# A fused attention and gated-MLP kernel: weight pieces are loaded before the first q and k, and their splitting is moved ahead

## The reference

```python
def _moe_ref(x, w1, w2, w3, w_out):
    a = x @ w1                      # 512 -> 1024
    b = x @ w2
    h = a * b @ w3                  # 1024 -> 1024
    return h @ w_out                # 1024 -> 512

def _moe2_ref(x, w1, w2, w3, w_out):
    h = np.maximum(np.maximum(x @ w1, x @ w2), x @ w3)   # 512 -> 768
    return h @ w_out                                     # 768 -> 512
```

## Time and profile before

| | us |
|---|---|
| median of 3 runs | 704.42 |
| lowest and highest run | 702.22, 706.07 |
| the profiled execution, whole | 706.01 |
| its span | 704.2 |
| TensorE busy in the span | 684.6 |
| mean granted TensorE clock | 0.995 |

### The profile page before, as it was taken

The page is one execution under the profiler, slowest core; times in us unless marked ns, Lnnn a source line. Parts: engine busy times, 40 slices in busy tenths (PEclk is TensorE's granted clock), DMA queues, the critical chain, the costliest instruction groups (busy, mean ns, idle before and its releaser), DMA issues.

```text
span 704.2 us, 15733 instructions
## 1 busy us (share of the span) xinstructions
PE 684.6 (97%) x6632; PEld 608.6 (86%) x6632; DVE 376.4 (53%) x705; ACT 242.2 (34%) x514; POOL 264.5 (38%) x241
## 2 busy tenths in 40 slices
PE   6999999999999999999999988999999999999998
PEld 4777788888888888888887988999999999999997
DVE  3464554414544044432665646566775667746673
ACT  5364432313332233333655544122341223403221
POOL 6799432312234023231222129043490434903341
PEclk9999999999999999999999998999999999999999
DMA  9874222111222022103998979876589765797632
GB/s 322 274 227 145 65 84 76 56 43 55 76 77 76 24 76 76 55 25 110 312 309 288 332 263 373 291 247 238 182 299 379 248 240 179 302 369 253 214 132 90
DMA packets 43798, 131.73 MB, mean 187 GB/s; under 512 B 4944, under 2 KB 8272, under 8 KB 42960
## 3 DMA queue, kind: packets, MB, share of 16 engines
q1 hardware_dynamic: 43728, 130.73, 53.7%
HBM read 103.97 MB, written 26.74 MB: 186 GB/s over the span
## 4 chain that ended last, share of the span: by engine, by line
PE 82%; DMA 6%; DVE 4%; POOL 3%; ACT 2%; issue 1%; SPq 1%; ACTq 0%; DVEq 0%
PE psum L585 25%; PE psum L587 24%; PE psum L586 24%; DMA weights_stream<-attention 4%; PE psum L624 2%; PE psum L602 2%; PE psum L595 2%; DVE attention L749 2%; POOL second_split L1147 2%; ACT attention L993 2%; DMA attention<-qk 2%; PE psum L612 1%; PE psum L633 1%; SPq L534 1%; DMA xy<-wa 1%
## 5 line engine op out<-in xcount | busy, mean ns | idle before, releaser
L585 PE MATMUL psum<-second_split,weights_split 128*128 128x384 f32 x402 | 135.7, 338 | 4.3 <-POOL second_split L1147 2.9
L586 PE MATMUL psum<-second_split,weights_split 128*128 128x384 f32 x402 | 134.9, 336 | 0.0
L587 PE MATMUL psum<-second_split,weights_split 128*128 128x384 f32 x402 | 134.9, 336 | 0.0
L1147 POOL TENSOR_TENSOR second_split<-xy,second_split 128x384 fp32r<-128x384 f32 x75 | 81.9, 1119 | 133.6 <-ACT second_split L993 133.6
L1147 POOL TENSOR_TENSOR h_split<-gate,h_split 128x512 fp32r<-128x512 f32 (+1 forms) x40 | 47.1, 1177 | 205.3 <-ACT h_split L993 205.3
L585 PE MATMUL psum<-x_split,weights_split 128*128 128x512 f32 (+1 forms) x320 | 120.4, 376 | 0.0
L587 PE MATMUL psum<-x_split,weights_split 128*128 128x512 f32 (+1 forms) x320 | 117.9, 369 | 0.0
L586 PE MATMUL psum<-x_split,weights_split 128*128 128x512 f32 (+1 forms) x320 | 117.9, 368 | 0.0
L585 PEld LDWEIGHTS psum<-second_split,weights_split 128*128 128x128 f32 x402 | 76.0, 189 | 6.6 <-issue 3.9
L586 PEld LDWEIGHTS psum<-second_split,weights_split 128*128 128x128 f32 x402 | 75.9, 189 | 0.0
L587 PEld LDWEIGHTS psum<-second_split,weights_split 128*128 128x128 f32 x402 | 75.9, 189 | 0.0
(11 more groups left out here) (101 smaller groups left out, 1152.5 us busy)
## 6 DMA issues: line engine op xcount, KB each, us to landing
weights_split<-weights_stream SPq DMA_DIRECT2D x39, 768.0 KB, 5.2
weights_split<-weights_stream SPq DMA_DIRECT2D x54, 512.0 KB, 5.0
weights_stream<-attention SPq DMA_DIRECT2D x48, 256.0 KB, 3.1
xy<-wa SPq DMA_DIRECT2D x40, 256.0 KB, 4.9
attention<-qk SPq DMA_DIRECT2D x16, 576.0 KB, 4.2
weights_stream<-attention SPq DMA_DIRECT2D x24, 384.0 KB, 2.8
weights_split<-weights_stream SPq DMA_DIRECT2D x6, 1152.0 KB, 5.0
attention<-v_win SPq DMA_DIRECT2D x16, 384.0 KB, 3.6
```

What stands on the lines that cost most here:

```text
L585: pe.matmul(out, lhs[:, 0], rhs[:, 0], start=first, stop=False, skip_group_check=read_between)
L586: pe.matmul(out, lhs[:, 0], rhs[:, 1], start=False, stop=False, skip_group_check=read_between)
L587: return pe.matmul(out, lhs[:, 1], rhs[:, 0], start=False, stop=last, skip_group_check=read_between)
L1147: return pool.tensor_tensor(out, full, high.bitcast(F32), ALU.subtract)
```

## The change

Seven edits, all in the first 40 us:

1. SyncE issues pieces 0 and 1 ahead of q and k of unit 0, then pieces 2 and 3 and the mask. Then it waits until q and k have landed, and issues the rest.
2. S of unit 0 moves behind step 3 of W3O, and T, V and S of the next unit follow: TensorE's order becomes steps 0 to 3, S, steps 4 to 10, T, steps 11 to 14, V, steps 15 and 16, S of unit 1, steps 17 to 23, T, steps 24 to 31, V. From there on the order is the old one.
3. Pieces 0 to 15 are split nine positions ahead of their slab's steps, not five. ScalarE therefore splits pieces 0 to 7 before the exponentials of unit 0, and pieces 12 and 13 before, 14 and 15 right behind those of unit 1. The positions at which pieces 12 to 27 are loaded stay as they were (`REFILL`), but q and k of unit 1 move with S of unit 0 and now stand behind pieces 16 and 17.
4. Steps 0 to 3 run term by term: four matmuls high by high, four high by low, four low by high, each term with its own wait.
5. The lows of pieces 1 and 3 are made by VectorE (`early_low`), with a semaphore of their own, and not by GpSimd.
6. VectorE fills 128 columns of `gate` with zeros, and TensorE multiplies them eight times (fp32, 128 columns) before step 0.
7. The semaphore on which TensorE and SyncE wait for a low of w3 is chosen by `wait_w3`.

```diff
-FIRST_VISITS = {"S": [-0.5, 15, 34.5, 47.5], "T": [7, 22, 40.7, 53.7], "V": [12, 31.9, 45.3, 58.3]}
+FIRST_VISITS = {"S": [3.5, 16.5, 34.5, 47.5], "T": [10, 23.5, 40.7, 53.7], "V": [14, 31.9, 45.3, 58.3]}
...
+EARLY = 2
+AHEAD, REFILL = 9, 5.5
...
-        out += [(4 * k - 5, ("SPLIT", 2 * k)), (4 * k - 4.9, ("SPLIT", 2 * k + 1))]
+        out += [(4 * k - AHEAD, ("SPLIT", 2 * k)), (4 * k - AHEAD + 0.1, ("SPLIT", 2 * k + 1))]
...
-    out = [(at + 1.5, ("PIECE", step[1] + SLOTS)) for at, step in weight_splits() if step[1] + SLOTS < PIECES]
+    out = [(at + (REFILL if step[1] < 2 * F1 else 1.5), ("PIECE", step[1] + SLOTS)) for at, step in weight_splits() if step[1] + SLOTS < PIECES]
...
-            load_qk(0)
             load_piece(0)
             load_piece(1)
+            load_qk(0)
             load_piece(2)
+            load_piece(3)
             sp.dma_start(mask, mask_in).then_inc(const_in, 16)
-            load_piece(3)
-            load_v4(0)
+
+            sp.wait_ge(qk_in, 16)
             load_piece(4)
             load_piece(5)
+            load_v4(0)
             sp.dma_start(ident, ident_in).then_inc(const_in, 16)
-            load_v(0)
             load_piece(6)
             load_piece(7)
+            load_v(0)
...
+            def first_product(i):
+
+                if i:
+                    return
+                high, both = (lambda i: w3_tile(0)[:, 0, P * i:P * (i + 1)]), w_out_tile(0)
+                pe.wait_ge(w_out_hi, 1)
+                pe.wait_ge(w3_hi, 1)
+                for i in range(4):
+                    pe.matmul(bank(i), high(i), both[:, 0], start=True, stop=False)
+                pe.wait_ge(w_out_lo, 1)
+                for i in range(4):
+                    pe.matmul(bank(i), high(i), both[:, 1], start=False, stop=False)
+                wait_w3(pe, 0)
+                for i in range(4):
+                    pe.matmul(bank(i), w3_tile(0)[:, 1, P * i:P * (i + 1)], both[:, 0], start=False,
+                              stop=False).then_inc(w3o_step, 1)
...
+            pe.wait_ge(zeros_made, 1)
+            for i in range(WARM):
+                pe.matmul(bank(7)[:, 0:P], gate[:, 0, 0:P], gate[:, 0, 0:P], start=True, stop=True)
...
+            def early_low(m):
+                dve.wait_ge(w3_hi, m + 1)
+                low(w3_tile(m)[:, 1, :], stage_a[2 * m + 1], w3_tile(m)[:, 0, :]).then_inc(w3_lo_early, 1)
+
+            dve.memset(gate[:, 0, 0:P], 0.0).then_inc(zeros_made, 1)
...
-                                 product_out(), after_parts("H"),
+                                 product_out(), after_parts("H"), [((-3.5, -2.5)[m], ("EARLY_LOW", m)) for m in range(EARLY)],
...
+            of_vector = [("SPLIT", 2 * m + 1) for m in range(EARLY)]
```

More of the change, by code:

```diff
@@ L48 @@
 SLOTS = 12
+WARM = 8
+EARLY = 2
+AHEAD, REFILL = 9, 5.5
 ATT = 6104
@@ L386, in build @@
         stage_a = [xy[:, T * (i // 3) + S + 512 * (i % 3):T * (i // 3) + S + 512 * (i % 3 + 1)] for i in range(SLOTS)]
-        const_in = sem("const_in")
+        const_in, zeros_made = sem("const_in"), sem("zeros_made")
         qk_in = sem("qk_in")
@@ L396, in build @@
         w_out_hi, w_out_lo = sem("w_out_hi"), sem("w_out_lo")
-        w3_hi, w3_lo = sem("w3_hi"), sem("w3_lo")
+        w3_hi, w3_lo, w3_lo_early = sem("w3_hi"), sem("w3_lo"), sem("w3_lo_early")
         w12_hi, w12_lo = sem("w12_hi"), sem("w12_lo")
@@ L426, in ge, with wait_w3 @@
                 eng.wait_ge(semaphore, value)
+        def wait_w3(eng, m):
+            if m < EARLY:
+                eng.wait_ge(w3_lo_early, m + 1)
+            else:
+                eng.wait_ge(w3_lo, m - EARLY + 1)
         def w3_tile(m):
@@ L496, in load_piece @@
                     elif kind == "w3":
-                        sp.wait_ge(w3_lo, n + 1)
+                        wait_w3(sp, n)
                     else:
@@ L635, in values @@
                 mm.then_inc(down_filled, 1)
+            def first_product(i):
[13 more added lines that the diff above has]
+                              stop=False).then_inc(w3o_step, 1)
             def product(half, k, i):
                 m = F1 * half + k
+                if m == 0:
+                    first_product(i)
+                    return
                 if i == 0:
-                    pe.wait_ge(w3_lo, m + 1)
+                    wait_w3(pe, m)
                     if half == 0:
@@ L859, in make_y @@
                 add.then_inc(y_made, 1)
-            run = {"qk_sum": qk_sum, "down_max": down_max, "local_max": local_max, "scale_down": scale_down,
+            def early_low(m):
+                dve.wait_ge(w3_hi, m + 1)
+                low(w3_tile(m)[:, 1, :], stage_a[2 * m + 1], w3_tile(m)[:, 0, :]).then_inc(w3_lo_early, 1)
+            dve.memset(gate[:, 0, 0:P], 0.0).then_inc(zeros_made, 1)
+            run = {"EARLY_LOW": early_low, "qk_sum": qk_sum, "down_max": down_max, "local_max": local_max, "scale_down": scale_down,
                    "scale_local": scale_local, "x_out": x_out, "W3O_OUT": product_low,
@@ L1183, in _ @@
                    "E": lambda e, kp: split_y(0, e, kp)}
-            for step in in_order(unit_jobs(["v_sum"]), weight_splits(), x_splits(), after_parts("H"),
+            of_vector = [("SPLIT", 2 * m + 1) for m in range(EARLY)]
+            for step in in_order(unit_jobs(["v_sum"]), [x for x in weight_splits() if x[1] not in of_vector],
+                                 x_splits(), after_parts("H"),
                                  [x for x in first_activations(0.4) if x[1][0] == "E"]):
```

## The result

The kernel after has a median of 706.53 us (702.66 to 707.93, 22 runs); the kernel before, run on the same chips, 703.38 us (702.22 to 707.72, 22 runs). The ratio is 1.0032 with a 95% interval of 1.0018 to 1.0045, some 2.3 us. (The means are 705.98 and 703.76, 2.2 apart; the medians lie 3.15 apart.) That is within the 0.5% that I called no change, but it is a small loss and not nothing. Its profiled execution has a span of 706.1 us (before 704.2) and a mean granted clock of 0.993. Neither profiled execution is a typical one: that of the kernel after, 707.93 us in all, is the longest of its 22, and that of the kernel before, 706.01, lies 2.6 above its median.

A forecast was written before the change was run, and what follows sets the result against it. TensorE, busy 684.6 of 704.2 us, was taken as the bound, leaving only its waits to gain. Landing later +2.5, shorter way -2.5 and clock +1.1 gave +1.1 us: median 705.5, range 701.3 to 707.6.

The forecast's parts named there:

- Step 0 near 5.4: Start of the kernel: piece 0 lands at 4.0, piece 1 at 4.8, so step 0 starts at about 5.4 us.
- rival 4: Start: piece 0 still takes 4.03 us, step 0 starts at 6.2, the end stays at 705.5; chance 0.07.
- q and k of unit 0 at 6.6: Start: this load, now third, lands at 6.6 us (range 6.0 to 7.4), just in time for S of unit 0.
- T of unit 0 with a wait of 1.4 at 16.4: Behind step 10: T can't start before some 16.4 us, TensorE is there at 14.9, a new wait of 1.4.
- q and k of unit 1 at 24.6, bounds 22.9 and 25.5: Load now behind pieces 16 and 17: leaves at about 14.6, lands at 24.6 us, 2.5 later than before.
- A wait of 3 to 4.5 before S of unit 1: TensorE, there at 23.0 or so, waits 3 to 4.5 us; S of unit 1 starts at 26.8.
- The issue wait goes: Scores of unit 1: TensorE's wait of 1.2 us for its own instructions probably goes, since S comes later.
- From S of unit 1 to step 28: 10.4 and 1.1 for the clock: This stretch takes 10.4 us, 12.93 before; one spell at half clock behind the long wait adds 1.1.
- The zeros are undone before S of unit 1: Eight zero matmuls at the start: by the skill's rule, the long wait before S of unit 1 undoes them.
- A shift passes to the end one to one: Behind the prologue everything is ordered behind TensorE, so a shift of the prologue reaches the end unchanged.
- Rival 2's cap: q and k of unit 1 not pushed back: step 28 up to 4.5 us earlier, 699.9 to 703.5; chance 0.23.
- Rival 3: SyncE's wait for the low of piece 5 makes q and k of unit 1 land after 27.0: 708 to 711; chance 0.07.

The follow-up runs named there:

- e2: Kernel after without SyncE's wait for q and k of unit 0; 706.14 us, ratio 1.0037 to the kernel before.
- e6: Kernel after without the matmuls of zeros; 705.04 us, ratio 1.0029 to the kernel before.
- e7: Kernel after with the lows of pieces 1 and 3 made by GpSimd, not VectorE; 705.22 us, ratio 1.0032 to the kernel before.
- e1: Kernel after with q and k of unit 1 issued right behind piece 11, ahead of pieces 12 to 17; 705.44 us, ratio 1.0026 to the kernel before.
- e10: e8 without the matmuls of zeros; 701.68 us, ratio 0.9971 to the kernel before.
- e12: e8 with q and k of unit 0 issued first again, ahead of pieces 0 and 1; 703.64 us, ratio 1.0004 to the kernel before.
- e8: Kernel after without SyncE's wait, q and k of unit 1 behind piece 11, pieces 12 and up held until V of unit 0 has run; 701.65 us, ratio 0.9978.
- e11: e8, but only pieces 12 to 15 go behind v of unit 1, the rest behind q and k of unit 2; 701.63 us, ratio 0.9971.
- e3: Kernel after without SyncE's wait and with q and k of unit 1 right behind piece 11; 704.28 us, ratio 1.0007 to the kernel before.
- e4: Kernel before with q and k of unit 1 issued right behind piece 11; 703.46 us, ratio 0.9994 to the kernel before.
- e9: Kernel before with q and k of unit 1 behind piece 11 and pieces 12 and up held until V of unit 0 has run; 702.77 us, ratio 0.9994.

## Why the prediction was right, and where not

The forecast, that q and k of unit 1 land later and eat the gain, holds by its main steps. I said 1.1 us slower; measured is 2.3 (1.3 to 3.2), so the size was too small by a factor of two. That the time itself, 706.53, comes near my 705.5 is in part luck: I started from a median of three runs, 704.42, and 22 runs of the same kernel give 703.38. Point by point:

- **Step 0 near 5.4.** It was 4.82. Piece 0 landed 2.7 us after its issue, not in the 4.03 that it had before; rival 4, no earlier step 0, is out. Both loads in one view (DMA issues of the kernel after, piece 0 and then piece 2):

```profile
xy<-wa SPq DMA_DIRECT2D x1, 256.0 KB, 2.7
...
xy<-wa SPq DMA_DIRECT2D x1, 256.0 KB, 6.9
```

- **q and k of unit 0 at 6.6.** This term was mis-sized, and the others hang on it. They landed at 8.3, since issued at 1.64 they took 6.66. My range ended at 7.4; in the other eight kernels that load them third they landed at 6.8 to 8.5, so the term also varies from one execution to the next. SyncE stands in its wait as long, so piece 4 left at 8.32 and not at 6.6, and the DMA engines were partly idle (windows; last numbers DMA share and GB/s):

```profile
6.00:8.00 2.00, 2.00 (x10) 1.64 (x9) 0.00 (x0) 0.00 (x0) 0.00 (x0) 1.00 0.67 241
...
8.00:10.00 2.00, 0.66 (x6) 0.27 (x6) 1.35 (x1) 0.96 (x2) 0.27 (x1) 1.00 0.41 113
```

  Before, the kernel moved 358 and 302 GB/s in the same two windows, and e2, without the wait, 321 and 353. S of unit 0 came at 9.73, not 8.1.
- **T of unit 0 with a wait of 1.4 at 16.4.** 1.1 at 17.87: the size is nearly right, the time late by 1.5, much of it the same gap.
- **q and k of unit 1 at 24.6, bounds 22.9 and 25.5.** It landed at 26.47 (25.6 and 26.9 in e6 and e7, whose loads are in the same order). The failed step is "2.5 us later"; it was 4.4, beyond my upper bound. The load left at 17.32 instead of 14.6: 1.7 of these 2.7 us because SyncE was released late, 1.0 because it took 9.0 us and not 8 for the 17 loads in front. It then took 9.15 and not 10. My bound took in the bytes in front, but not that q and k of unit 0, and with them SyncE, could be late. e2 puts a figure on SyncE's wait: without it, landing at 25.1, 1.4 earlier. The rest is the position in the order: e1 lands at 20.4 with the wait left in, though in that execution SyncE was also released 1.4 us earlier.
- **A wait of 3 to 4.5 before S of unit 1.** 3.87.
- **The issue wait goes.** It did in unit 1, because S is now later than the block: the packet landed at 27.29, and the scores only start at 29.55. In e1, where they start at 24.47, its packet landed at 26.75 and they waited.
- **From S of unit 1 to step 28: 10.4 and 1.1 for the clock.** 40.24 less 28.66 = 11.58, against 11.5. By e7's 10.17 at the full clock the way was 0.2 shorter and the spell, 1.4 us, 0.3 longer than worked out. Only the start was wrong, so step 28 lay outside my 36.5 to 38.5: 3.0 us later than before where the sum had 1.1.
- **The early lows cost nothing.** They took 1.25 and 1.22 us each, the 1.3 that I took, beside GpSimd's work, and e7, at the same ratio of 1.0032, shows no worth either way.
- **The zeros are undone before S of unit 1.** e6 and e10 show no change of the total without them (1.0029 and 0.9971). That they are lost in the wait before S of unit 0 (1.34 in the kernel after, none in e6) was not in my text. The Trainium skill (TensorE: Matmul & The Clock Gate, Why this matters for your kernels) has long idle gaps bring the low clock back. By that rule the 3.9 us wait costs a second warm-up. The trace agrees there.
- **A shift passes to the end one to one.** In the medians it does: +3.2 at the MLP's start, +3.15 in the median, +2.2 in the mean; and over all the kernels to within 1.3 us. e2, 1.9 us earlier at the MLP than the kernel after and no faster, and e12 (0.9 earlier than before, 1.0004) are the widest misses. In the profiled pair it doesn't show: +3.0 at step 28, +3.2 at the MLP's start, +1.6 at 422, +0.2 at 431, +2.6 from 445 on, +1.9 at the end. This is the sign of being wrong that I had named, waits behind 40 us that come or go with their slow spells at 423 and 436: the first was missing in the kernel after, the second longer. One execution of each kernel can't carry this step.
- **Rival 2's cap.** I had priced an early landing at up to 4.5 us before, with "the issue wait off". e1 made the landing early and refutes this: the issue wait comes back as 3.10 us and brings the slow spell with it. In the kernel as it stands the rival was worth nothing that the times show (1.0026); with SyncE's wait out and the queue short it comes to 1.5 to 2.0 us against the kernel before (e8 0.2%, e11 0.3%).
- **Rival 3**, q and k landing after 27.0, was missed by 0.5 us: its price would have come in from there, though what made the load late was in good part the gap, as e2 shows, and no low of piece 5 was needed for it.

So the gain of the early start went in two places, one behind the other: the load of q and k of unit 1, pushed behind pieces 16 and 17 and held up by SyncE's wait, and, as soon as that is mended, TensorE's own instructions, which come over the same DMA engines.

## What to carry to other kernels

When a load is given precedence, write down the issue time of every load that is moved behind it and of the load that a queue's wait stands on; here the one load whose release moved with another edit took the whole gain. A stall named "issue" under heavy DMA traffic is a load too: find the instruction at which it stops, see whether it stays there when the start is shifted, and keep the queue short around it rather than moving matmuls; the packets on the instruction queue tell when the block was fetched. Give the same landmark in every profile by the same instruction, and don't read a total of 0.3% from one profiled execution of each kernel: here the stretch between the MLP's start and 430 us alone moved by 3 us between executions of kernels that are the same there. And when a wait is removed without effect, look for the next one at the same place before calling the removed one harmless.

## What the hardware showed that I had not expected

- TensorE's instructions can be late by 1.2 to 3.1 us while the pieces load, always at the same place, behind 705 records or 512 and 1024 more. TensorE goes on 1.4 to 1.5 us after a packet of 16 KB has landed on the instruction queue, and with the DMA engines full of pieces that packet begins 2.5 to 4.9 us after TensorE is 256 records ahead of the border, with a short queue 0.9 to 1.5.
- In e6 the second group of four matmuls takes 1.71 us, 0.43 each, where the kernel after needs some 0.23, and the windows from 5 to 9 us still read a granted clock of 1.00. At the start of a kernel the record doesn't show the slow pace; the pitch of the matmuls does.
- The same 576 KB of q and k take 5.1 to 6.9 us behind two pieces (nine kernels), 8.0 to 10.8 in the full queue, and piece 2, right behind them, takes 6.9 where piece 0 takes 2.7.
- Waits of 3.9 (the kernel after), 3.1 (e1, e2, e6), 2.4 (e3), 2.2 (e7, before T of unit 0) and 2.0 us (e8, before S of unit 0) were each followed by a granted clock of 0.50, as was the one of 2.1 at 420 before. Not every wait of that length was: one of 2.1 us at 417.6 in e10 left the clock at 1.00. The waits of 1.5 us and less (e4, e7, e9, e11) all did. So did the waits before the first matmuls, up to 6.1 us, where the record doesn't show the pace anyway.
